# Wider stationary tiles for the state update, and a new hand-written order of tasks, in an attention and two-layer MoE kernel on one core

## The reference

```python
def _attn_ref(r, k, v, w, u):                 # B, H, S, D = 4, 8, 768, 48
    state = zeros((B, H, D, D))
    for t in range(S):
        cur = einsum('bhd,bhe->bhde', u[None] * k[:, :, t], v[:, :, t])
        y[:, :, t] = einsum('bhd,bhde->bhe', r[:, :, t], state + cur)
        state = w[:, :, t, :, None] * state + einsum('bhd,bhe->bhde', k[:, :, t], v[:, :, t])
    return y

x = attn(...)                                 # as 3072 tokens x 384
h = maximum(maximum(x @ w1, x @ w2), x @ w3)  # 384 -> 768
x2 = h @ w_out                                # 768 -> 384
l = x2 @ w_in                                 # 384 -> 1024
e = exp(l - max(l)); sm = e / (sum(e) + 1e-9)
z = l * sm
out = ((z - mean(z)) / sqrt(var(z) + 1e-6) * g_ln) @ w_out2   # 1024 -> 384
```

## Time and profile before

| what | value |
|---|---|
| median of 3 runs | 776.59 us (776.34 to 777.71) |
| the profiled execution | 776.59 us, its span from first to last instruction 774.8 us |
| busy share of the span | PE 94%, PEld 78%, DVE 64%, ACT 38%, POOL 9% |
| granted TensorE clock | 2.4 GHz nearly all the time from 80 us on, partly 1.2 GHz between 20 and 94 us |

### The profile page before, as it was taken

One profiled execution on the slowest core, in us unless ns is written; L12 is line 12 of the kernel. 1 busy time (PEld: TensorE's weight loads), 2 busy tenths in 40 slices (PEclk: granted clock), 3 DMA queues, 4 the chain that ended last, 5 costly groups with the idle time before them and its releaser, 6 DMA issues.

```text
span 774.8 us, 21949 instructions
## 1 busy us (share of the span) xinstructions
PE 727.5 (94%) x9280; PEld 604.1 (78%) x9280; DVE 494.7 (64%) x944; ACT 296.4 (38%) x698; POOL 72.9 (9%) x178
## 2 busy tenths in 40 slices
PE   4776999999999999999999999999999999999987
PEld 3666778778887778888878888877988877888776
DVE  5998666698455688566589566578665568222381
ACT  4434432674313445132447123336233236211260
POOL 2222301201011101011010011010110100000000
PEclk9956899999999999999999999999999999999999
DMA  7345523155222045420134511216611004400043
GB/s 243 114 129 172 178 87 107 32 152 177 89 79 78 5 126 178 128 78 20 60 109 148 178 51 43 64 42 186 186 45 40 2 7 135 130 10 1 1 136 121
DMA packets 56706, 74.92 MB, mean 97 GB/s; under 512 B 8224, under 2 KB 43296, under 8 KB 56608
## 3 DMA queue, kind: packets, MB, share of 16 engines
q1 hardware_dynamic: 56192, 73.44, 30.0%
q10 hardware_dynamic: 416, 0.08, 0.1%
HBM read 48.58 MB, written 22.54 MB: 92 GB/s over the span
## 4 chain that ended last, share of the span: by engine, by line
PE 78%; DVE 9%; issue 3%; DMA 3%; SPq 2%; ACT 1%; DVEq 0%; ACTq 0%
PE ps L608 17%; PE ps L609 15%; PE ps L610 15%; PE ps L667 14%; PE ps L564 10%; PE ps L585 3%; PE ps L603 3%; DVE z_blocks L869 2%; DVE rk_sb L804 2%; PE ps L594 1%; DMA z_turning<-z_blocks 1%; DMA zT<-z_turning 1%; DVE e_sb L909 1%; DVE neg_max L903 1%; DVE scoresT L825 1%
## 5 line engine op out<-in xcount | busy, mean ns | idle before, releaser
L667 PE MATMUL ps<-w_moe_out,zT 128*128 128x384 f32 x384 | 132.9, 499 | 8.5 <-ACT out_sb L782 4.8
L804 DVE TENSOR_TENSOR rk_sb<-rk_sb,decay 112x512 f32<-112x512 f32 x144 | 97.6, 698 | 54.4 <-PE ps L564 53.6
L608 PE MATMUL ps<-xT,w_moe 128*128 128x512 f32 x324 | 131.0, 404 | 0.3 <-issue 0.3
L667 PEld LDWEIGHTS ps<-w_moe_out,zT 128*128 128x128 f32 x384 | 118.5, 315 | 15.3 <-issue 6.0
L609 PE MATMUL ps<-xT,w_moe 128*128 128x512 f32 x324 | 126.9, 392 | 0.0
L610 PE MATMUL ps<-xT,w_moe 128*128 128x512 f32 x324 | 126.7, 391 | 0.0
L564 PEld LDWEIGHTS ps<-rk_sb 48*64 48x64 f32 x4224 | 86.0, 148 | 50.7 <-issue 34.2
L564 PE MATMUL ps<-rk_sb 48*64 48x32 f32 (+1 forms) x4224 | 98.2, 233 | 20.4 <-DVE rk_sb L804 16.9
L709 ACT COPY scoresT<-ps 16x128 f32<-16x128 f32 (+2 forms) x168 | 55.8, 333 | 87.5 <-PE ps L564 78.5
L752 ACT CAST h_x<-e_sb 128x512 fp32r<-128x512 f32 x36 | 22.4, 621 | 173.9 <-DVE e_sb L888 173.9
L832 DVE COPY_PREDICATED scoresT<-level_m,ps 64x256 f32<-64x256 uint32 x144 | 76.6, 532 | 4.0 <-PE ps L564 1.4
(11 more groups left out here) (78 smaller groups left out, 953.8 us busy)
## 6 DMA issues: line engine op xcount, KB each, us to landing
rk_sb<-in_rk SPq DMA_DIRECT2D x24, 512.0 KB, 4.2
z_turning<-z_blocks SPq DMA_DIRECT2D x24, 512.0 KB, 3.2
zT<-z_turning SPq DMA_DIRECT2D x96, 128.0 KB, 2.9
w_sb<-in_w SPq DMA_DIRECT2D x24, 224.0 KB, 4.0
k_turning<-k_blocks SPq DMA_DIRECT2D x20, 256.0 KB, 2.3
k_tok<-k_turning SPq DMA_DIRECT2D x80, 64.0 KB, 2.2
v_sb<-in_v SPq DMA_DIRECT2D x24, 192.0 KB, 4.2
out<-out_sb SPq DMA_DIRECT2D x24, 192.0 KB, 2.1
```

What stands on the lines that cost most here:

```text
L608: nc.tensor.matmul(o, a[0], b[0], start=first, stop=False)
L667: last = nc.tensor.matmul(ps[:, OUT, 0:DM], zT[:, t % 2, :, c], w_moe2_out[:, c, :], start=(c == 0), stop=(c == J2 - 1))
L804: nc.vector.tensor_tensor(both, both, by, ALU.mult).then_inc(scaled, 1)
```

## The change

Three things change together.

1. `k_tok` gets the layout [token, feature, pair] in place of [token, block of 32, pair, 32]. The DVE transpose writes `k_blocks` with elements four apart (16 bytes) instead of next to each other. The DMAs keep their sizes. The update reads 64 stationary columns of `k_tok` with a step of four elements, in 8 matmuls instead of 16.
2. Two waits go: in `exps` one on `var_done`, in `norm` one on `scale_done`. Both wait for earlier work of the same engine.
3. The four order strings are rewritten.

```diff
 START = """
-    a0 0 b0 0 b1 a1 0 1 0 1 0 a2 1 0 1 0 1 0 1 M z z b2 v z q 1 2 2 p 1 2 M v z a3 2 q 3 2 3 p 2 b3 3 2 3 2 3 M z z a4
-    v q 3 4 3 4 3 p b4 b5 4 z z M q p v z 4 a5"""
+    b0 a0 0 a1 0 1 b1 0 1 0 0 1 a2 0 1 0 1 0 z 1 M 2 z 1 b2 q v p 2 1 2 z z z M v z a3 2 3 2 3 q b3 p 2 3 2 3 2 b4 3 M
+    v a4 q 3 4 3 4 3 4 p 4 b5 z z M q p a5 z v"""
...
-        k_tok = sb("k_tok", [128, BLOCKS, PAIRS, BL])
+        k_tok = sb("k_tok", [128, BLOCKS * BL, PAIRS])
...
-                        sp.dma_start(k_tok[b * BL:(b + 1) * BL, :, :, :].rearrange("p a q d -> p a (q d)"),
+                        sp.dma_start(k_tok[b * BL:(b + 1) * BL, :, :].rearrange("p (a d) q -> p a (d q)", a=BLOCKS),
...
-                        for a in range(BLOCKS):
-                            i = a * BL // HB
-                            last = nc.tensor.matmul(upd[a * BL:(a + 1) * BL, q * D:(q + 1) * D], k_tok[:, a, q, :],
+                        for i in range(2):
+                            last = nc.tensor.matmul(upd[i * HB:(i + 1) * HB, q * D:(q + 1) * D], k_tok[:, i * HB:(i + 1) * HB, q],
...
-                    act.wait_ge(var_done, 4 * m + (t - 1))
...
-                    nc.vector.transpose(k_blocks[:].rearrange("p (b q j) -> p b q j", b=BLOCKS, q=PAIRS),
+                    nc.vector.transpose(k_blocks[:].rearrange("p (b j q) -> p b q j", b=BLOCKS, q=PAIRS),
...
-                    if m or i:
-                        dve.wait_ge(scale_done, 2 * m + i)
```

More of the change, by code:

```diff
@@ L59 @@
 START = """
-    a0 0 b0 0 b1 a1 0 1 0 1 0 a2 1 0 1 0 1 0 1 M z z b2 v z q 1 2 2 p 1 2 M v z a3 2 q 3 2 3 p 2 b3 3 2 3 2 3 M z z a4
-    v q 3 4 3 4 3 p b4 b5 4 z z M q p v z 4 a5"""
+    b0 a0 0 a1 0 1 b1 0 1 0 0 1 a2 0 1 0 1 0 z 1 M 2 z 1 b2 q v p 2 1 2 z z z M v z a3 2 3 2 3 q b3 p 2 3 2 3 2 b4 3 M
+    v a4 q 3 4 3 4 3 4 p 4 b5 z z M q p a5 z v"""
 FIRST = """
-    . . . . . z u00 u01 . . u02 u10 M v z . z u11 . . d0 u12 . . u20 u21 . . y d1 u22 . . u30 d2 M v . . u31 z u32 u40
-    z . . u41 z u42 z u50 g u51 z . . z d3 u52 . q g . d4 d5 . l0 p q e0 p x0 c0 l1 M t0 v e1 x1 q l2 c1 e2 . . h0 t1
-    h1 n00 x2 g n01 g l3 n02 c2 . . e3 o0 t2 n03 x3 p w0 c3 . . h2 n10 t3 o1 w1 M h3 v n11 n12 q n13 . p o2 w2 . . o3
+    . z . . z . u00 u01 g . z . u02 u10 . . u11 u12 d0 z M v . . u20 u21 g . . z z u22 d1 . . u30 y u31 d2 u32 . . g
+    u40 d3 u41 M v u42 . . u50 z z u51 u52 q . . z d4 d5 p . . q l0 . e0 . g x0 l1 p . M c0 e1 t0 q x1 v l2 c1 . n00 h0
+    t1 e2 . x2 p n01 l3 c2 h1 . n02 . n03 o0 t2 e3 w0 x3 c3 . . h2 t3 o1 M w1 h3 v q n10 n11 n12 . o2 n13 p . . w2 o3
     w3"""
 STEADY = """
-    . . u00 u01 . . u02 u10 . . u11 M v . . d0 u12 u20 . . u21 u22 d1 . . y u30 u31 . . d2 M v . . u32 u40 u41 . . u42
-    u50 . . d3 u51 u52 d4 q . p . d5 . q l0 e0 M v x0 . c0 t0 p l1 e1 . x1 h0 l2 c1 . t1 e2 h1 n00 x2 n01 q c2 l3 t2
-    n02 n03 . o0 e3 x3 p w0 . c3 h2 . t3 o1 M h3 w1 v . q n10 o2 n11 n12 p n13 w2 . . o3 w3"""
+    . . u00 u01 . . u02 u10 . . u11 u12 d0 M v . . u20 u21 u22 u30 . y . u31 d1 . . u32 u40 . . d2 M v . . u41 u42 u50
+    . . u51 d3 . . u52 d4 q . . p d5 . q l0 M p v e0 x0 . c0 t0 l1 q e1 . x1 p l2 h0 c1 . e2 t1 n00 x2 l3 c2 n01 h1 .
+    t2 n02 o0 e3 n03 w0 x3 h2 . c3 . t3 o1 n10 w1 M h3 v q n11 p n12 . n13 o2 w2 . . o3 w3"""
 LAST = """
-    u00 u01 u02 u10 u11 d0 u12 u20 u21 u22 u30 u31 d1 d2 u32 u40 u41 u42 u50 u51 d3 u52 d4 d5 l0 e0 x0 c0 l1 t0 h0 e1
-    x1 l2 c1 e2 t1 l3 x2 e3 c2 h1 o0 n00 x3 t2 c3 h2 n01 n02 n03 t3 n10 n11 n12 n13 w0 o1 h3 w1 o2 w2 o3 w3"""
+    u00 u01 u02 u10 u11 u12 u20 d0 u21 u22 u30 d1 u31 u32 d2 u40 u41 u42 u50 u51 d3 u52 d4 d5 l0 e0 x0 l1 c0 e1 t0 x1
+    c1 h0 l2 e2 t1 x2 h1 l3 n00 c2 n01 e3 t2 n02 o0 n03 w0 x3 h2 c3 t3 n10 o1 w1 n11 h3 n12 o2 n13 w2 o3 w3"""
 def slot_order():
```

## The result

The changed kernel takes 795.7 us (median of 4 runs, 792.5 to 797.35) against 776.55 us: a ratio of 1.0239, 95% interval 1.0205 to 1.0272, so 19.1 us slower. The direction was forecast, the size was not: 786.5 us, at most 789.5. The profiled execution is the longest of its kind, 798.28 us with a span of 796.4; its lines show where time goes, while the sum is made on the medians of the experiments.

The account below looks back on a forecast made before the run. PE was taken as the bound in STEADY (118.55 of 120 us busy), DVE in START. Terms 8.5 + 1.5 + 1.4 - 1.9 + 2.4 = +11.9 gave 788.5 us; less 2, 786.5; range 773.5 to 789.5.

Parts of the forecast that it names:

- The step: State update on PE: reading 64 columns 16 bytes apart lengthens the block to 0.97 us; +8.5 us, bounds -0.2 and +8.5.
- the 8-byte and the 32-byte row: Profile rows around the unseen 16-byte step: 8 bytes nearly free, 32 bytes 0.98 ns a column; the 32-byte price was taken.
- The same at the lower clock: Three updates in START: step price doubled to 1.0 us each, half taken as DVE covers part; +1.5 us, bounds 0 and +3.
- START: Order from the kernel's start to the first large matmul: shorter DVE wait and one slot fewer; -1.9 us, bounds -4 and +1.
- The transpose of k: DVE transpose goes from 699 to 699 or 1048 ns; only the four in START count, +1.4 us, bounds 0 and +1.4.
- DVE's free third covers it: In the large-matmul stretches, DVE's idle third was said to hide the transpose's extra 0.35 us.
- the discount: 2 us taken off the total because the block's and the transpose's prices stood at their upper bounds.
- now a slot stands between, and most of that goes: START, behind the first mix: DVE's 1.03 us wait for ACT's rounding of a weight chunk mostly vanishes, -1.0 us.
- FIRST: Stage after START: slots move from its `u` part into its logits part, where DVE is fullest; 0, bounds +-2 us.
- Splits spread better: In FIRST, better-spread splits were named alongside the moved slots in the term given 0.
- STEADY: Three stretches: repacks ahead of the `zT` load and a later weighing cost +0.8 each; +2.4 us, bounds -1 and +5.
- The tail and the two removed waits: LAST's order almost kept, nothing counted as won, bounds -1 and +1 us; removed waits on engines' own finished work, 0.

Follow-up runs that it names:

- adjacent columns: Kernel before with the new layout and 8 matmuls of 64 columns, reading neighbouring (wrong) columns, old orders, against the kernel before: 780.53 us, ratio 1.0052.
- the layout alone: Kernel before with the new `k_tok` layout, transpose and 8 matmuls of 64 columns, old orders and both waits kept, against the kernel before: 785.38 us, ratio 1.0117.
- One such edit: Kernel before with two slots moved ahead of `b2 v z q` behind START's first mix, against the kernel before: 779.39 us, ratio 1.0029.
- the two runs of the orders: Kernel before with the four new order strings, without and with the two waits removed, against the kernel before: 790.4 us (ratio 1.0181) and 786.86 us (1.0147).

## Why the prediction was off

**The step: right.** Forecast 0.97 us for the block at the full clock, measured 0.99; the loads read 214 ns where "near 190" was said. +8.5 for 17 blocks is 8.7 (17 times 0.51). The choice between the 8-byte and the 32-byte row fell on the right one.

**The same at the lower clock: too dear.** I doubled the price to 1.0 us and took half. The three blocks of START last 0.965, 0.991 and 0.991 us against 0.80: +0.5 in all, forecast +1.5. The step's price is not doubled with the clock; it nearly goes. With adjacent columns the same blocks last 0.89 us, so the step costs 0.10 there and 0.49 at the full clock.

**The transpose of k: right in size, wrong on the cover.** 1112 ns for the forecast 1048. "DVE's free third covers it" is false: the slot behind the mix waits for the state's addition, which the transpose holds up. In the layout alone the wait is not there since the slow block lets PE come later; with adjacent columns it is 2.6 of +4.0. For START, where +1.4 was forecast, no effect can be told from the spread of START.

Together the layout terms were +11.4, or 9.4 with the discount; measured 8.8 (7.5 to 10.6). That the sum came out so near has some luck in it: the block's term was right, of the 2.9 us of the other two the trace shows 0.5, and the 2 taken off for another reason made up for the rest.

**START: the step that failed.** Forecast -1.9 with bounds -4 and +1, and a first large matmul between 79 and 82 us; it starts at 86.31, and the new START alone is +7.6. The sentence "now a slot stands between, and most of that goes" is where it broke. I read the 1.03 us as a wait that any instruction in between would fill, and did not ask what the slot's mask itself waits for: PE's slot, queued behind the mix. One such edit cost 2.3 us where -1.0 was forecast, shown by experiment; the moved `z` cost about another 2 by the second update. The wait at the end, worth about 2 of its 4.95 us, I did not see at all, since the trace of before has no row for a `z` and POOL's multiplication right ahead of the state's part. Rows show what stands in it (ACT's rounding late by 2.2, then DVE's 1.95 us beside POOL), but moving `v` won only 1.1 us there; it is not settled whether another order would spare it.

**FIRST: given 0 with bounds of 2; alone it is +5.0.** "Splits spread better" had no row, and the profiled execution of it alone holds only 1.1 of the 5.0. In the changed kernel FIRST is 2.6 us longer without its four blocks, with two stretches at 1.2 GHz in it. What makes the rest of the 5.0 stays open. DVE is busy 19.1 of 20 us between 160 and 180 us before, so slots moved there could hardly do anything but wait.

**STEADY: right mechanism, term too small.** The lateness of `zT` was forecast at 0 to 0.9 us a stretch, 0.5 taken; the waits measure 1.1 to 1.6 in the changed kernel. The stretches themselves, without their four blocks each, are longer by 0.3, 2.3 and 1.0 us where 0.8 each was forecast, and the 2.3 hold the stretch at 1.2 GHz: most of the excess is the clock. I followed SP's queue to the load, and not DVE's second transpose, which waits 0.76 for z's store. The wait before the fourth `l` was to be 1.2 us and is 0.87 as before. STEADY with LAST is +4.9 against +2.4, within the term's bound of +5.

**What no term held.** A wait of PE can be followed by 3.5 us at 1.2 GHz, 1.3 to 1.7 us each time, four times in the profiled execution. With 5 to 7 us it is as large as the error of START. The rows before had none behind a wait, so waits were priced at their length. What decides whether the clock falls behind a wait stays open.

**The tail and the two removed waits: 0**, as forecast as far as the runs can tell. LAST takes 97.1 and 97.0 us in the two runs of the orders against 97.2; the +1.3 of the changed kernel is the clock. The premise was not quite right: `d0`, `d1` and `d2` change places among the `u` of LAST.

The range ended at 789.5 since the priced step was joined to order terms near zero. With the upper bounds of the order terms as I had written them (START +1, STEADY +5, FIRST +2, tail +1) it would have reached 788.5 + 2.9 + 2.6 + 2 + 1 = 797; they were not carried into the range, and that is a fault of the working beside the one of START.

## What to carry to other kernels

On an engine in order, a wait is filled only by an instruction that has its own inputs by then: before a slot is moved into a wait, look up what the slot waits for. In an order with slack of a fraction of a us, every move costs, and sums of separate moves say little; price such a change by the whole bound, and test it in halves. A stationary operand read with a step of 16 bytes costs about 1 ns a column at 2.4 GHz in a block with 48 moving columns; 8 bytes cost next to nothing. Look at the granted clock behind every new wait of PE before the loss is put down to the order of tasks.
